# Issue order of the first attention loads: at most three under way

## The reference

```python
for c in range(nc):                       # chunks of 32 queries
    k_full = [mem_k (8), k from 16 before the chunk to 8 behind it]
    v_full = the same of v
    scores = scale * q_c @ k_full.T
    a = softmax(scores)
    out[:, :, chunk] = a @ v_full
```

## Time and profile before

| | |
|---|---|
| median of 3 runs | 743.81 us |
| the runs | 740.81, 743.81, 744.53 us |
| the profiled execution's own time | 740.97 us |
| its span (first to last instruction) | 739.2 us |
| TensorE busy | 699.6 us, 95% |
| VectorE, ScalarE, GpSimd busy | 514.2, 329.0, 321.6 us |
| mean granted TensorE clock | 0.961 |
| moved by DMA | 89.09 MB, 121 GB/s on the mean |

### The profile page before, as it was taken

The page is one execution under the profiler, slowest core; times in us unless marked ns, Lnnn a source line. Parts: engine busy times, 40 slices in busy tenths (PEclk is TensorE's granted clock), DMA queues, the critical chain, the costliest instruction groups (busy, mean ns, idle before and its releaser), DMA issues.

```text
span 739.2 us, 18078 instructions
## 1 busy us (share of the span) xinstructions
PE 699.6 (95%) x7190; PEld 624.6 (84%) x7190; DVE 514.2 (70%) x1945; ACT 329.0 (45%) x540; POOL 321.6 (44%) x242
## 2 busy tenths in 40 slices
PE   7999973899999999999999999999999999999992
PEld 5999962798899889988998899889988998999881
DVE  4577776787888688868876888688768886451240
ACT  1455546432681357135713571357135713571360
POOL 2111126881772277227622762276227622762011
PEclk8799985799999999999999999999999999999997
DMA  8999994601330233023302330223022302320001
GB/s 320 327 374 380 395 380 158 227 2 58 101 114 30 71 101 115 30 72 101 115 29 75 98 114 30 75 96 114 30 80 94 114 29 82 106 99 30 0 15 43
DMA packets 24925, 89.09 MB, mean 121 GB/s; under 512 B 3360, under 2 KB 3360, under 8 KB 24864
## 3 DMA queue, kind: packets, MB, share of 16 engines
q0 software_dynamic: 13056, 46.14, 19.0%
q1 hardware_dynamic: 11808, 42.17, 15.2%
HBM read 75.71 MB, written 12.58 MB: 119 GB/s over the span
## 4 chain that ended last, share of the span: by engine, by line
PE 94%; DVE 2%; issue 1%; DMA 1%; ACT 0%; POOL 0%; DVEq 0%; POOLq 0%; ACTq 0%
PE banks L606 26%; PE banks L608 24%; PE banks L607 24%; PE banks L512 3%; PE banks L491 3%; PE banks L635 3%; PE banks L462 3%; PE bank L473 2%; PE bank L503 2%; PE banks L619 1%; PE bank L599 1%; PE bank L532 1%; PE bank L539 1%; DMA gath<-x_rows,ids 1%; DVE hot_b L1151 0%
## 5 line engine op out<-in xcount | busy, mean ns | idle before, releaser
L1497 POOL TENSOR_TENSOR wl<-raw,wh 128x1024 fp32r<-128x1024 f32 x60 | 146.8, 2448 | 30.3 <-ACT wh L836 29.2
L1491 POOL DMA_INDIRECT raw<-w,w_idx x60 | 66.3, 1105 | 147.7 <-DVE w_idx L1201 107.9
L606 PE MATMUL banks<-xh,wh 128*128 128x384 f32 x256 | 90.5, 354 | 2.0 <-DVE xl L1342 2.0
L606 PE MATMUL banks<-hh,wh 128*128 128x384 f32 x256 | 90.2, 352 | 0.0
L608 PE MATMUL banks<-xh,wl 128*128 128x384 f32 x256 | 86.4, 337 | 0.0
L608 PE MATMUL banks<-hh,wl 128*128 128x384 f32 x256 | 86.2, 337 | 0.0
L607 PE MATMUL banks<-xl,wh 128*128 128x384 f32 x256 | 86.1, 336 | 0.0
L607 PE MATMUL banks<-hl,wh 128*128 128x384 f32 x256 | 85.8, 335 | 0.0
L606 PE MATMUL banks<-wout_h,uh 128*128 128x512 f32 x192 | 79.0, 411 | 0.0
L606 PE MATMUL banks<-win_h,yh 128*128 128x512 f32 x192 | 77.4, 403 | 0.0
L608 PE MATMUL banks<-wout_h,ul 128*128 128x512 f32 x192 | 75.4, 393 | 0.0
(11 more groups left out here) (212 smaller groups left out, 1577.1 us busy)
## 6 DMA issues: line engine op xcount, KB each, us to landing
unit<-qk_in SPq DMA_DIRECT2D x24, 768.0 KB, 6.6
vr<-v_in SPq DMA_DIRECT2D x24, 520.0 KB, 5.8
x_rows<-x_keep SPq DMA_DIRECT2D x20, 256.0 KB, 5.3
prep_early<-w_in SPq DMA_DIRECT2D x2, 512.0 KB, 7.5
x_rows<-x_sb SPq DMA_DIRECT2D x4, 256.0 KB, 5.1
prep_first<-w_in SPq DMA_DIRECT2D x2, 512.0 KB, 5.8
prep_first<-w_out SPq DMA_DIRECT2D x2, 512.0 KB, 7.3
prep_rest<-w_out SPq DMA_DIRECT2D x2, 512.0 KB, 8.8
```

Source lines behind the costliest of these rows:

```text
L606: nc.tensor.matmul(bank, stat_h, mov_h, start=first, stop=False)
L1491: gp.indirect_dma_start(stage(s, c), None, table, bass.IndirectOffsetOnAxis(ap=w_idx[:, c % WCH:c % WCH + 1], axis=0))\
L1497: gp.tensor_tensor(wl[:, c % WCH, :], stage(s, c), wh[:, c % WCH, :].bitcast(F32), ALU.subtract)\
```

## The change

Before its loop SyncE issues the loads in another order, and six of them only after an earlier load has landed (the wait is on that load's semaphore). The waits that stand in `load_qk` and `load_v` themselves stay. The loop, all other engines, the buffers and the sizes are the same.

```diff
             load_qk(1)
             load_v(0)
+            sp.wait_ge(qk_loaded[0], 16)
+            load_qk(2)
+            sp.wait_ge(qk_loaded[1], 16)
             load_v(1)
-            for u in range(2, DEEP):
-                load_qk(u)
-                load_v(u)
+            sp.wait_ge(v_loaded[0], 16)
+            load_qk(3)
+            sp.wait_ge(qk_loaded[2], 16)
+            load_v(2)
+            sp.wait_ge(v_loaded[1], 16)
             load_qk(DEEP)
+            sp.wait_ge(qk_loaded[3], 16)
+            load_v(3)
             for u in range(NT - DEEP):
```

## The result

In 19 executions each, the changed kernel took 745.96 us at the median and the kernel before 742.70; the ratio is 1.0039 with a 95% interval of 1.0026 to 1.0053. The change makes the kernel 0.39% slower. One of the 19 executions of the changed kernel took 1717 us and is left out of the ratio. The prediction was 743.3 us and a gain of 0.5 us. The time is just inside the range given, within 0.5% of before, and on the other side of zero. The spread says the same: of all executions in this record, 96 of 171 of the kernel before and 7 of 42 of the changed one took under 743 us.

A forecast was written before the change was run, and what follows sets the result against it. TensorE was taken to bound the kernel, 94% of the span. Loads cost or gain TensorE 0, the code block gains 0.5 us: 740.97 - 0.5 = 740.5, carried to the median 743.3 us; range 739.5 to 746.

The forecast's parts named there:

- The issue times: SyncE's six held loads before the loop: issues at about 5.3, 8.2, 9.7, 11.7, 13.1 and 15.1 us.
- The first term: TensorE's first code block, hole of 2.33 us near 11 us: fewer open loads shorten it, 0.5 us taken as gain.
- the bound below nothing: TensorE's code block in the first 26 us: gain between nothing and the whole hole, 2.33 us; no loss expected.
- it should stay there: DMA engines before the loop: share 1.00 at 11.10 and 0.98 until 18.3 us, to stay so with two loads waiting.
- bubbles between loads: Six landing waits: engines empty 1.0 us each lose 6 us, giving 745.7 us; at 2.0 us each 751.7; chance 0.08.
- the clock staying up: TensorE's first 26 us: code block early enough, clock might not fall; gain 2.5 to 4.1 us, 741.3 to 739.7; chance 0.18.
- The Trainium skill's rule: Code block on the DMA engines: with packet-by-packet turns, load queue depth doesn't matter; sum 0 instead of 0.5 us.

The follow-up runs named there:

- shifted kernel: Kernel before with two warm-up matmuls instead of three and ten tiny ones behind them, so loop instructions stand 36 later in TensorE's program; 1.0022 (0.9997 to 1.0047).
- order alone: Changed kernel without its six landing waits, only the new order of loads; 1.0011 (0.9987 to 1.0034) to the kernel before.
- first three waits: Changed kernel with only the first three of its six landing waits (holding unit 2, values 1 and unit 3); 1.0018 (1.0002 to 1.0035).
- waits alone: Kernel before in its old load order, with a landing wait ahead of each of the last six loads; 1.0047 (1.0023 to 1.0071).
- second comparison: Changed kernel, unaltered, measured again against the kernel before; 1.0016 (0.9991 to 1.0041).
- three comparisons: The three measurements of the unaltered changed kernel against the kernel before; 1.0039, 1.0016 and 1.0034.
- one load at a time: Changed kernel's new order, with each load held until the one ahead has landed; 1.0181 (1.0143 to 1.0219) to the kernel before.
- shorter loads: Kernel before with the q/k loads of units 1 to 5 at half their columns, 384 of 768 KB; 0.9966 (0.9944 to 0.9989).
- two under way: Changed kernel's new order with at most two loads under way instead of three until values 3 have gone out; 1.0000 (0.9978 to 1.0022).
- last three waits: Changed kernel with only the last three of its six landing waits (holding values 2, unit 4 and values 3); 1.0021 (1.0001 to 1.0041).
- quiet start: New order; values 0 await unit 0, unit 2 unit 1, values 1 and unit 3 unit 2, values 2 values 1, rest free; 0.9973, then 0.9993 to the kernel before.

## Why the prediction was wrong

**Right.** The issue times came within 0.9 us, unit 2 landed at 11.6 us, and TensorE never waited for a load. From unit 6 to the end the traces take 705.2 us before and 705.4 in the changed kernel on the mean of three, though single ones lie up to 2.6 us apart. The thing in reach was TensorE's code; the shifted kernel shows that the holes are just that. The first term came out near as a number: the first hole shrank from 2.48 to 1.83 us on the mean of three traces, 0.65 against the 0.5 us that I took. Half of that is luck. The packet begins 0.34 us sooner (11.15 to 10.81); the rest is that TensorE starts the value block 0.3 us later (10.09 to 10.40), which is due to the third trace.

**Wrong: the bound below nothing.** I wrote, "A loss isn't to be expected, since the loads open are never more than now." This is the step that failed: the code block's term had nothing as its bound on the side of a loss. It looked at the first block and at the number of open loads. The second packet begins 1.8 to 2.1 us after TensorE goes on behind the first hole in the kernel before, and 3.0 to 4.3 us after it in the changed one; the third begins at 22.4 to 22.5 instead of 20.5 to 22.6. Before, SyncE issues no load from 8.7 to 13.8 us, and the DMA share from 14 to 16 us, when the second block is fetched, is 0.93, 0.87 and 0.88; in the changed kernel, where fresh loads follow each landing, it is 0.99, 0.96 and 0.97. That fuller engines are why the block is later is only argued. The order alone fits it (1.03, packet 3.3 us after); with the first three waits it is 0.78 there and 1.01 from 16 to 20 us, and the packet comes only at 19.0.

**Wrong: "it should stay there".** The prediction kept the DMA engines as full as before. From 0 to 20 us they move 298 GB/s instead of 317 on the mean of three traces, 0.4 MB less. No load was late for it, so what it costs isn't shown.

**Wrong: the size of what hangs on it.** The holes sum to the same in both kernels (3.2 and 3.0 us on the mean). What differs between the two sets of traces is the clock. From 8 to 38 us the mean of 0.74 before and 0.66 after means 2 x 30 x 0.08 = 4.8 us more at the low level; each of them costs 1 - 3.41/5.58 = 0.39 of its length, so 1.9 us. Start to unit 6 is longer by 31.5 - 29.8 = 1.7 us. The accounting holds: six steps at the high clock (6 x 3.41 = 20.5 us), the holes, and 0.39 of the time at the low level give start to unit 6 in each of the six traces within 0.4 us.

The link from late blocks to the clock is not shown. Three traces of the kernel before spread over 3 us by themselves, more than the 1.7 us. With the order alone the second block is late and the clock returns early. With the waits alone and with the first three, the clock from 8 to 38 us is 0.77, as in the first trace of before, and the loss stands in the holes, 5.0 and 6.0 us. And over all executions (42 and 152 whose clock is on record) the mean granted clock is 0.9583 against 0.9602, which is 2.9 us more at the low level, at most 1.1 us of the 2.6 by which the mean span is longer; in the second comparison the clock isn't lower at all.

The three comparisons give 0.39, 0.16 and 0.34%, about 2.2 us. The holes behind the loop (near 103 us; 0.58, 0.52, 0.30 before, 1.12, 0.52, 0.99 after) would be 0.4 of it, which no experiment tested. I had the clock in a rival, but only as something to win.

**The rivals.** The rival on the slower side, bubbles between loads, isn't what happened in the way it was priced: fewer bytes were moved early, but GpSimd had 3.2 us of slack or more and no load was waited for. Only with one load at a time did TensorE wait, 1.0181. There unit 1 takes 3.98 us from its issue to that of the next load and values 0 take 3.24; with 2.0 and 1.4 us of moving at the rates of the earlier trace rows that leaves 1.8 to 2.0 us empty at each, where the prediction took 1.0. The faster rival, the clock staying up, occurred in the kernel with shorter loads (0.9966, or 2.5 us, with an interval of 0.8 to 4.2), so its price of 2.5 to 4.1 us fits. The Trainium skill's rule, "DMA: Bandwidth & Descriptors", section on queues, rings and completion order, that engines take turns packet by packet gave a sum of 0 by my reading, since the depth of the queue would not matter. In these runs it does: the first packet begins at 8.6 to 9.7 us with at most two loads under way and at 10.9 to 12.2 with free issue. No trace shows when the block is asked for, so it stays open whether the turn-taking or the asking differs.

**Open.** Why a block arrives when it does, and what carries the rest of the loss beyond the clock. The number of open loads explains the first block and not the later ones with two under way (2.71 and 0.96 us of holes). Halving the rows didn't change it. The trace shows neither when a block is asked for nor on which DMA engine it waits.

## What to carry to other kernels

In the first pass through this long loop the DMA view lists TensorE's instructions (queue 8) beside the loads: look for holes put down to "issue" that end 1.2 to 1.7 us after a code packet has ended, and see that packet as a transfer with a due time of its own. Don't judge a change in issue order by whether loads are in time; compare packet times and granted clock over several traces, since two traces of one kernel differed by more than the two kernels. Then test the account that comes out of the traces against the clock and time of all executions: here the clock covers less than half of the loss.

## What the runs showed of the hardware that I had not expected

A 16 KB code block took 0.9 to 1.5 us to move before 30 us, and TensorE went on 1.2 to 1.7 us after its end. In five of the six traces of the two kernels a second hole of 0.5 to 2.1 us stood between 18 and 25 us, and in those five the clock was back at 2.4 GHz for good only at 32.1 to 37.6 us; in the one without it, at 26.2. (With the order alone and with the last three waits, also without it, the clock was back before 30 us.) Three holes of 0.5 to 1.06 us at the high clock, with the shorter loads, didn't bring it down to 1.2 GHz; in the quiet start's first trace it fell behind a single one of 1.10 us. Loads in rows of 1536 and 1040 bytes moved 343 GB/s from 26 to 96 us at a full share, against 376 with rows four times as long.
